# The opening of a fused attention and two-layer expert kernel: ScalarE order, one scaling step moved to VectorE, key loads ahead of two weight loads, value loads spread

## What is computed

```
# 1 attention, per batch and head (8 heads of 64); q is 576 x 64
k_p, v_p = k, v averaged over groups of 8 tokens          # 72 keys
scores = q @ k_p.T / 8;  scores -= scores.max(-1)
attn = exp(scores); attn /= attn.sum(-1) + 1e-9
x = attn @ v_p                                            # heads side by side: 4608 x 512
# 2 dense layer pair
h = x @ w_in                                              # 512 -> 2048
g = max(h, 0) + alpha * min(h, 0)
y = g @ w_out                                             # 2048 -> 512
# 3 each token goes to the one of 8 experts whose embedding is nearest (cosine / tau, softmax gate)
out[token] = gate * (max(y @ w1[e], 0) @ w2[e])           # 512 -> 1024 -> 512
```

## Time and profile before

| | |
|---|---|
| median of 3 runs | 1475.15 us |
| the profiled execution: its own time, its span | 1475.51 us, 1473.8 us |
| TensorE matmul busy | 1452.0 us, 99% of the span |
| VectorE, ScalarE, GpSimd busy | 779.8, 498.9, 658.2 us |
| granted TensorE clock, mean | 0.995 |

### The profile page before, as it was taken

The page is one execution under the profiler, slowest core; times in us unless marked ns, Lnnn a source line. Parts: engine busy times, 40 slices in busy tenths (PEclk is TensorE's granted clock), DMA queues, the critical chain, the costliest instruction groups (busy, mean ns, idle before and its releaser), DMA issues. The chain is left out here.

```text
span 1473.8 us, 22006 instructions
## 1 busy us (share of the span) xinstructions
PE 1452.0 (99%) x7773; PEld 1197.1 (81%) x7773; DVE 779.8 (53%) x1498; ACT 498.9 (34%) x869; POOL 658.2 (45%) x622
## 2 busy tenths in 40 slices
PE   8999999999999999999999999989999999999998
PEld 7888878888888888888888888868888888888886
DVE  7666676676767676766566576840002700064640
ACT  3333322232232322222322212634444444444442
POOL 5552243253252342432322333465555755566662
PEclk9999999999999999999999999999999999999999
DMA  8534131131131221311110221441112511035310
GB/s 251 154 119 145 38 106 51 38 99 44 46 119 29 70 82 38 98 43 30 44 49 9 65 79 58 158 157 44 44 42 94 198 52 44 32 111 184 109 59 12
DMA packets 67336, 119.53 MB, mean 81 GB/s; under 512 B 9756, under 2 KB 26140, under 8 KB 67104
## 3 DMA queue, kind: packets, MB, share of 16 engines
q1 hardware_dynamic: 59200, 99.20, 21.3%
q0 software_dynamic: 8032, 18.93, 4.0%
HBM read 92.34 MB, written 29.43 MB: 83 GB/s over the span
## 5 line engine op out<-in xcount | busy, mean ns | idle before, releaser
L1588 POOL TENSOR_TENSOR g_lo<-g_full,g_hi 128x512 fp32r<-128x512 f32 x144 | 192.7, 1338 | 516.7 <-ACT g_hi L1360 516.5
L757 PE MATMUL h_ps<-x_hi_in,weight_parts 128*128 128x512 f32 x1144 | 376.5, 392 | 0.0
L773 PE MATMUL y_ps<-weight_parts,g_hi 128*128 128x512 f32 x1152 | 361.0, 395 | 0.9 <-issue 0.9
L1360 ACT ACTIVATE g_hi<-g_full 128x512 fp32r<-128x512 f32 x144 | 91.1, 632 | 519.7 <-PE y_ps L773 410.1
L773 PEld LDWEIGHTS y_ps<-weight_parts,g_hi 128*128 128x128 f32 x1152 | 213.9, 189 | 46.5 <-issue 1.5
L757 PEld LDWEIGHTS h_ps<-x_hi_in,weight_parts 128*128 128x128 f32 x1144 | 215.0, 188 | 43.8
L879 PE MATMUL y_ps<-weight_parts,x_hi_in 128*128 (+1 forms) x1032 | 244.3, 393 | 3.0 <-POOL x_hi_in L1639 3.0
L879 PEld LDWEIGHTS y_ps<-weight_parts,x_hi_in 128*128 128x128 f32 x1032 | 195.1, 189 | 44.6 <-issue 3.2
L773 PE MATMUL y_ps<-weight_parts,g_lo 128*128 128x512 f32 x576 | 225.5, 392 | 0.0
L757 PE MATMUL h_ps<-x_lo_in,weight_parts 128*128 128x512 f32 x572 | 223.1, 390 | 0.0
L1046 DVE TENSOR_SCALAR g_full<-h_ps,alpha 128x512 f32<-128x512 f32 x144 | 107.6, 747 | 218.1 <-PE h_ps L757 217.5
(11 more groups left out here) (198 smaller groups left out, 1703.7 us busy)
## 6 DMA issues: line engine op xcount, KB each, us to landing
shared<-in_w SPq DMA_DIRECT2D x8, 2048.0 KB, 8.7
emb_all<-in_w SPq DMA_DIRECT2D x8, 2048.0 KB, 8.9
y_dram<-y_rows SPq DMA_DIRECT2D x9, 1024.0 KB, 4.3
shared<-in_q SPq DMA_DIRECT2D x34, 256.0 KB, 2.9
shared<-in_v SPq DMA_DIRECT2D x29, 288.0 KB
x_dram<-shared SPq DMA_DIRECT2D x32, 256.0 KB, 3.3
y_rows<-x_dram SPq DMA_DIRECT2D x32, 256.0 KB, 3.6
shared<-in_k SPq DMA_DIRECT2D x26, 288.0 KB, 2.8
```

The source lines that it names most:

```text
L757: mm = pe.matmul(h_ps[:, f % 2, :], w[:, k, f * P:(f + 1) * P], x[:, k, :], start=(n == 0), stop=(n == 3 * DC - 1))
L773: mm = pe.matmul(y_ps[:, j, :], a[:, f % 2, j * P:(j + 1) * P], w[:, f, :], start=(f == 0 and n == 0), stop=(f == FC - 1 and n == 2))
L1360: act.activation(gh[:, f % 2, :], g_full[:, f % 2, :], ACT.Copy).then_inc(gh_done, 1)
L1588: pool.tensor_tensor(gl[:, f % 2, :], g_full[:, f % 2, :], gh[:, f % 2, :].bitcast(F32), ALU.subtract).then_inc(gl_done, 1)
```

## The change

It has four parts, all in the front and in tile 0:

- ScalarE: `exps(3)` stands ahead of `copy_turned(1)`, and `w_hi(0)`, `w_hi(1)` ahead of both; `w_hi(2)` and `w_hi(3)` stand ahead of `first_x_hi(0)` and of `copy_turned(2)`.
- The scaling of step 3, `norm(3)`, is taken from GpSimd and written out on VectorE, right behind `row_scale(3)`; TensorE's 8 filler transposes between `values(1)` and `turn_probs(3)` are left out.
- SyncE issues weights 0 and 1, then keys 4 to 7, then weights 2, queries 4, values 4 and weights 3.
- `v_at(0, f)` gives value chunks 4, 5, 6, 7 at f = 0, 2, 3, 4 (before: 0, 1, 2, 3). The reductions and the loads of the next chunk follow it.

```diff
         def v_at(i, f):
-            if i == 0 and f < PAIRS:
-                return PAIRS + f
+            if i == 0 and f in (0, 2, 3, 4):
+                return PAIRS + max(f - 1, 0)
...
-            for n in range(4):
+            for n in range(2):
                 load_w(n)
-            load_k(PAIRS)
-            load_k(PAIRS + 1)
+            for n in range(PAIRS, 2 * PAIRS):
+                load_k(n)
+            load_w(2)
             load_q(4)
-            load_k(PAIRS + 2)
-            load_k(PAIRS + 3)
             load_v(PAIRS)
+            load_w(3)
...
             values(1, h_ps[:, 1, :])
-            keep_busy(WARM // 4, y_ps[:, 0, 0:P])
             turn_probs(3)
...
             row_scale(3)
+            dve.wait_ge(recip_done, 4)
+            dve.wait_ge(normed, 3)
+            dve.tensor_tensor(prob[:, 1, :, :], prob[:, 1, :, :],
+                              rs[:, 1, :].unsqueeze(2).to_broadcast([QB, HEADS, KEYS]), ALU.mult).then_inc(normed, 1)
             w_lo(1)
...
             exps(2)
-            copy_turned(1)
-            exps(3)
             w_hi(0)
             w_hi(1)
+            exps(3)
+            copy_turned(1)
+            w_hi(2)
+            w_hi(3)
             first_x_hi(0)
             copy_turned(2)
-            w_hi(2)
             first_x_hi(1)
             copy_turned(3)
-            w_hi(3)
             first_x_hi(2)
...
             w_lo(0)
-            norm(3)
             w_lo(2)
```

## The result

| | before | after |
|---|---|---|
| median of 20 runs each | 1475.91 us | 1478.49 us |
| lowest, highest | 1473.86, 1479.15 | 1474.68, 1483.90 |
| ratio, 95% interval | | 1.0021 [1.0012, 1.0031] |
| profiled execution, its span | 1475.51, 1473.8 | 1477.33, 1475.6 |
| start of the first product of tile 0 | 29.14 us | 32.52 us |

The change makes the kernel 0.21% slower, about 3 us, where 1475.6 (0.45 us more than before) was forecast; 1478.49 lies just above the range. (The 20 runs of before have a median 0.76 us above that of the first three.) Five of the 20 runs after took 1482 us or more, all five at a mean granted clock of 0.990 or 0.991; the slowest of before took 1479.15.

A forecast was written before the change was run, and what follows sets the result against it. TensorE, busy 99% of the span, was taken as the bound. A later start of tile 0 (+1.35 us) and a removed gap (-0.90) gave +0.45 on the median 1475.15: 1475.6 us, range 1472.4 to 1478.3.

The forecast's parts named there:

- rival 2: Front, TensorE: its clock falls after 3.3 us of idling, giving 1477.3 or up to 1479.0 us; chance 0.32.
- the sum: Whole kernel: +1.35 us for the late start of tile 0, -0.90 for the values, +0.45 us in all.
- The idle time: TensorE in the front, from the end of `turn_probs(3)` at 24.0 until `values(2)` at about 27.3: 3.3 us.
- the earlier trace that priced the rival: Profile before: after 2.2 us idle near 220 us, a 3.41 us stretch at clock 0.50, priced at 1.7 us.
- Inside a wait and off the path: TensorE's 8 filler transposes ahead of `turn_probs(3)`: they lay inside a wait, so removing them was given no cost.
- The late weights: Front, ScalarE: weights 3 land at 25.2 behind the other loads, so tile 0 starts at 30.5, +1.35 us.
- the bound above, 25.5: Latest landing of weights 3, 0.63 us ahead of where weights 4 landed before; it would make the start +1.65 us.
- 5.24: Microseconds from the start of `w_hi(3)` on ScalarE to the first product of tile 0.
- The values: Tile 0, batch 1: value chunk 5 asked for at f = 2 removes TensorE's gap ahead of 50.33, -0.90 us.
- Below that there is no idle time to take: Limit on the gain from the value chunks: from 0 to -0.90 us, no more.
- The scaling chain: Front, step 3: scaling on VectorE takes 0.75 us, `turn_probs(3)` starts at 22.95, 2.2 us earlier, hidden behind ScalarE.

The follow-up runs named there:

- after_again: The kernel after once more, unchanged, timed on the same chip as the kernel with 36 transposes; ratio 1.0013 to the kernel before.
- after_fill8: The kernel after with the 8 identity transposes between `values(1)` and `turn_probs(3)` put back; ratio 1.0014 to the kernel before.
- filler36: The kernel after with 36 identity transposes on TensorE between `turn_probs(3)` and `values(2)`; ratio 1.0003 to the kernel before.
- no_filler: The kernel before without the 8 identity transposes between `values(1)` and `turn_probs(3)`; ratio 1.0005 to the kernel before.
- filler: The kernel after with 24 identity transposes on TensorE between `turn_probs(3)` and `values(2)`; ratio 1.0011 to the kernel before.
- keys_only: The kernel before with only SyncE's new order of loads; ratio 0.9995 to the kernel before.
- splits_only: The kernel before with only `w_hi(2)` and `w_hi(3)` moved early on ScalarE, as in the change; ratio 0.9997 to the kernel before.
- spread_only: The kernel before with only the value chunks of batch 1 taken at f = 0, 2, 3, 4; ratio 0.9986 to the kernel before.
- split_back: The kernel after with `w_hi(2)` and `w_hi(3)` back where they stood before, loads still in the new order; ratio 0.9977 to the kernel before.
- loads_back: The kernel after with SyncE's loads issued in the old order, all else still changed; ratio 0.9998 to the kernel before.

## Why the prediction was wrong

- **What failed: rival 2 was not in the sum.** The idle time was forecast as 24.0 to 27.3 us and came as 24.4 to 28.1; but the sum had no term for it: the fall of the clock stood at nothing in the forecast and was given 0.32 of the chances. The reason given against it, that bursts of work lie close on both sides, does not hold: in the traces of after, after_again and after_fill8 the clock fell each time, for 6.8 us, twice the stretch of the earlier trace rows that priced the rival. By filler36 against after_again it is worth about 1.4 us, by the clock of the runs (after_again 0.0019 below before, at 1.45 us for 0.001) 2.8. The section "Why this matters for your kernels" of the page "TensorE: Matmul & The Clock Gate" of the Trainium skill, which speaks for this outcome, was quoted and then left at a third; the trace after agrees with it (3.72 us idle, then 6.83 us at 0.50).
- **The 8 transposes were priced at nothing.** "Inside a wait and off the path" is true of their time and false of what they do: no_filler has a clock 0.0018 lower. In the kernel after they were not the whole of it: with them back (after_fill8) TensorE still idled 3.13 us and the clock still fell in the trace.
- **The late weights: right mechanism, size too small.** Weights 3 were put at 25.2 with `w_hi(3)` at 25.25. It started at 26.07, 26.50, 26.98 and 27.78 in the traces of after, after_fill8, after_again and filler; the bound above, 25.5, taken from the spacings of one trace, was no bound. Two slips lie beside it. 16.11 is where the last of the four issues of L539 starts, not where they end (6.60 + 9.84 = 16.44); the landing at 20.1 is right all the same. And the sum took 0.75 for keys and queries whose spacing it had just read as 0.8; with 0.8 it gives 25.5. The first product of the trace after at full clock would have come at 26.07 + 5.24 = 31.3, or 2.2 us late, not 1.35; some of that may be the trace's own, as the fronts of keys_only and splits_only were 0.7 to 0.8 us late from their `copy_turned(1)` on. Over the runs, with the clock whole (filler36, +0.4 us by means) and the values' 1.9 us taken off, the late start costs about 2.3, whatever the filler itself costs included; at equal clock (0.7 us below before, values taken off) it is about 1.2.
- **The values: right in kind, perhaps larger.** -0.90 forecast, -1.9 measured with a standard error of 0.55. The gap ahead of L773 went as forecast. "Below that there is no idle time to take" fails in the one trace of spread_only, where the wait of L801 in tile 1 is 1.2 us shorter; in the other twelve traces with the spread values it is 0 to 0.8 shorter. Where the second microsecond comes from, if it is real, stays open. (The gap ended at 50.33 when the first of GpSimd's two `w_lo` was done, 48.95 + 1.27, not the second at 51.4 as the prediction says; its size is the same.)
- **The scaling chain: right to a few tenths.** `turn_probs(3)` at 22.95 forecast, 23.36 seen, scaling 0.75 and 0.76; its gain was hidden behind ScalarE, as said.
- **Together:** by the fillers -1.9 + 2.3 + 1.4 = +1.8 us, by the clock of the runs -1.9 + 1.2 + 2.8 = +2.1 us, beside 1.9 (0.0013) and 3.1 (0.0021) measured. That each sum comes out is no test of its terms, since the late start was got as what is left over. The split between late start and clock rests on overlapping intervals and stays open within more than 1 us. What is settled is the cause behind both: `w_hi(2)` and `w_hi(3)` ahead of the copies while their weights come late.

## What to carry to other kernels

Two edits that are each free can spend the same slack: before a load is moved back in a queue, look at what now stands behind the instruction that needs it, and undo one of the two. Filler on TensorE inside a wait has a price when it is taken out, and it isn't its own duration: look at the granted clock of many runs, not at one trace (the one trace of split_back has a half-clock stretch in the front, and over its ten runs the clock is that of before). Where an engine gets work from another, ask what that other one does at the same moment.

## What the runs showed of the hardware

- The clock can fall after less idle time than the 3.7 us seen in the kernel after. In the front of no_filler it fell with no wait of TensorE over 2.29 us, in loads_back with none over 1.68, in split_back with none over 1.40. The work just before was alike in amount: in loads_back 2.19 us of matmuls in 3.41, mostly `values` of 72 rows, and the clock fell; in the kernel before 2.17 us in 3.42, half of them the filler transposes, and it stayed at 1.00. In none of the eight traces with the 8 transposes there and waits of 1.3 us at most behind them did it fall in this part of the front.
- VectorE beside a GpSimd subtraction of 128x512: a 128x8 operation took 1.27 us instead of 0.17, a 128x576 product 1.54 instead of 0.76.
- The same transfer at the same place in the queue, weights 3, took 9.5 us from issue to landing in one trace of the kernel after and 10.4 in another (after_again); filler and split_back had 10.9 and 11.3. ScalarE could start on it at 26.07, 26.98, 27.78 and 28.84; in split_back 1.0 us of that is a later issue. That is scatter of the size of the whole effect.
